# Moving TensorE's operands by 32 bytes: loaded tensors on multiples of 64, streamed ones on 32 modulo 64

## The chip, the cores and the metric

The kernel runs on one core of a Trainium2 chip. The metric is the device time of one execution in microseconds (us), median of several runs.

## The reference

Sliding-window attention with a few global keys, then two feed-forward networks over the same 1,536 tokens. All tensors are float32.

```python
# attention: batch 2, 8 heads, 768 positions, head size 64; 8 global keys, 96 local ones
keep = (key < n_global) | ((rel >= 0) & (rel < n_local))
scores = where(keep, q @ k.T / sqrt(64) - slope[h] * dist, -1e9)
x = softmax(scores) @ v                      # -> (1536, 512)
# first feed-forward network: 512 -> 1024 -> 512
h = x @ w_in
x = (layernorm(h * softmax(h)) * g_ln) @ w_out
# second one: 512 -> 1536 -> 512
xn = x / rms(x) * rms_g
out = (silu(xn @ w_gate) * (xn @ w_val)) @ w_down
```

## The kernel before

One program, five engines, every wait written out by hand with semaphores. The work has two parts.

In the first part a loop goes over 12 tiles of 128 tokens. For each tile the four head pairs are scored (`score_pair`), the probabilities are turned (`turn_pair`) and multiplied with the values (`mix_pair`). Between these the first feed-forward network of the tiles before is worked in: `turn_x`, `ffn_in`, `turn_ln`, `ffn_out`.

In the second part a loop goes over 6 blocks of 256 tokens. Each block has 12 steps, m = 0 to 11. A step is `widen` for the gate columns (12 matmuls), `widen` for the value columns (12 matmuls), and `narrow` for the step before (6 matmuls). At m = 7 and m = 10 a `turn_y` of four transposes for the next block stands between gate and value.

Each product of two float32 tensors is made of three matmuls in the type float32r, over a rounded part `_hi` and the rest `_lo` of each factor (lines 396, 397, 398, which in the trace carry all of these products):

```python
def product(pe, acc, hi, lo, other_hi, other_lo, first, last):
    pe.matmul(acc, hi, other_hi, start=first, stop=False)
    pe.matmul(acc, hi, other_lo, start=False, stop=False)
    return pe.matmul(acc, lo, other_hi, start=False, stop=last)
```

The second argument of a matmul is loaded into TensorE as weights (always 128 or 116 columns), the third is streamed through it. So `widen` loads the weight matrices `gate` and `val` and streams the activations `yt`; `narrow` loads the activations `act` and streams the matrix `down`; `ffn_in` loads `xt` and streams `in`; `ffn_out` loads `ln` and streams `out`. A transpose loads the tensor that it turns and streams `ident`. `mix_pair` loads `probs_t` and streams `v_in` in plain float32; the transposes too are plain float32. The load of one matmul goes on while the matmul before it streams.

The matrices lie in blocks of 512 columns. Blocks 0, 1 and 2 of `gate` and `val` serve the steps m = 0 to 3, 4 to 7 and 8 to 11; the blocks of `down` serve `narrow` of the same m.

Where a tensor lies: `sbuf` (line 94) takes the next address in every partition that is a multiple of 32 bytes, in the order of the calls. The first tensor, `ident`, starts at byte 16,512, a multiple of 64. Most sizes are multiples of 64 bytes, so a tensor has the residue of the one ahead of it, until a small tensor shifts it. Tensors of the second part lie over those of the first part. Added up from the shapes, the start of each tensor that TensorE reads is, modulo 64 (inside a tensor every slice that a matmul of float32r starts at, except the keys and probabilities, adds a multiple of 64):

| matmuls | loaded: residue | streamed: residue |
|---|---|---|
| `widen`, blocks 0 and 2 | gate, val: 0 | yt: 32 |
| `widen`, block 1 | gate, val: 32 | yt: 32 |
| `narrow`, block 0 | act: 32 | down: 32 |
| `narrow`, block 1 | act: 32 | down: 0 |
| `narrow`, block 2 | act: 32 | down_hi: 32, down_lo: 0 |
| `ffn_in` | xt: 0 | in: 32 |
| `ffn_out` | ln: 0 | out: 0 |
| `mix_pair` | probs_t: 32 | v_in: 32 |
| `score_pair` | queries in qk_hi: 32 | keys in qk_hi, k_lo: 32 for one head, 0 for the other |
| `turn_pair` | probs: 32, 48, 0, 16 in turn | ident: 0 |
| `turn_x`, `turn_ln` | x, gated: 0 | ident: 0 |
| `turn_y` | yn: 32 | ident: 0 |

Of the kernel before, what the change touches and what calls it, by code (L numbers as in the profile page):

```python
# [23 lines left out]
F32 = mybir.dt.float32  # L24
# [3 lines left out]
P = 128  # L28
# [6 lines left out]
FAR = 1 << 20  # L35
BATCHES = 2
SPARE = 8192
RSQRT_SEED = float(0x5F3759DF)
NEWTON = 3


def fused_kernel(nc, qk_pairs, v_windows, n_global, n_local,
# [47 lines left out]
    with whole:  # L90
        def sem(name):
            return whole.enter_context(nc.semaphore(name))

        def sbuf(ctx, name, shape, dt=F32):
            return ctx.enter_context(nc.sbuf_tensor(name, shape, dt))

        w_hi, w_lo = {}, {}

        def place(ctx, keys):
            for kind, n in keys:  # L100
                w_hi[kind, n] = sbuf(ctx, f"{kind}{n}_hi", [P, KJ, BANK], F32R)
                w_lo[kind, n] = sbuf(ctx, f"{kind}{n}_lo", [P, KJ, BANK], F32R)


        ident = sbuf(whole, "ident", [P, P])
        gln_col = sbuf(whole, "gln_col", [P, K1])
        rms_col = sbuf(whole, "rms_col", [P, KM])
# [8 lines left out]
        with ExitStack() as one:  # L116
# [4 lines left out]
            v_in = sbuf(one, "v_in", [HALF, 2, 2, model])  # L121
# [17 lines left out]
            in_front_of_spare = nc.sbuf_bytes_remaining  # L139
            spare = sbuf(one, "spare", [P, SPARE])  # L140

# [5 lines left out]
            for name, width in widths.items():  # L147
                gen[name] = spare[:, at:at + width]
                at += width
            assert at <= SPARE  # L150
            x = sbuf(one, "x", [P, heads, d])
# [19 lines left out]
        with ExitStack() as two:  # L171
            place(two, plan[OVER_ATTENTION:OVER_IN])
            y_in = sbuf(two, "y_in", [P, 2, 2, model])
            yn = sbuf(two, "yn", [P, 2, model])
            yt_hi = sbuf(two, "yt_hi", [P, 2, KM, WIDE], F32R)
            yt_lo = sbuf(two, "yt_lo", [P, 2, KM, WIDE], F32R)
            silu = sbuf(two, "silu", [P, 2, WIDE])
            act_sb = sbuf(two, "act_sb", [P, 2, WIDE])
            act_hi = sbuf(two, "act_hi", [P, 2, WIDE], F32R)
            act_lo = sbuf(two, "act_lo", [P, 2, WIDE], F32R)  # L180
            o_sb = sbuf(two, "o_sb", [P, 2, model])

            place(two, [plan[OVER_ATTENTION - 1]])
            kind, n = plan[-1]
            w_hi[plan[-1]] = sbuf(two, f"{kind}{n}_hi", [P, KJ, BANK], F32R)
            sbuf(two, "unused", [P, (nc.sbuf_bytes_remaining - in_front_of_spare) // 4])

            place(two, plan[FFN2:OVER_ATTENTION - 1])
            place(two, plan[OVER_IN:-1])
            w_lo[plan[-1]] = sbuf(two, f"{kind}{n}_lo", [P, KJ, BANK], F32R)  # L190
# [612 lines left out]
        def _(dve):  # L803
# [204 lines left out]
            def take_variance(t):  # L1008
# [13 lines left out]
                dve.wait_ge(ln_steps, at + 8)  # L1022
                nc.vector.tensor_scalar(seed_bits[:, 1:2], seed_bits[:, 0:1], -1.0, RSQRT_SEED,
                                        ALU.mult, ALU.add).then_inc(seed_ready, 1)
# [12 lines left out]
            def scale_of_y(b):  # L1037
# [3 lines left out]
                if not known(b) or b >= 1:  # L1041
# [6 lines left out]
                dve.wait_ge(rms_steps, at + 2)  # L1048
                nc.vector.tensor_scalar(rstd_bits[:, 1], rstd_bits[:, 0], -1.0, RSQRT_SEED, ALU.mult, ALU.add
                                        ).then_inc(rms_steps, 1)  # L1050
# [403 lines left out]
```

## Time and profile before

| | before |
|---|---|
| median of 3 runs | 599.11 us (598.56 to 600.3) |
| span of the profiled execution (its own time is not listed apart from it) | 596.7 us |
| TensorE matmul busy | 566.4 us, 95% |
| VectorE busy | 305.0 us, 51% |
| ScalarE busy | 258.1 us, 43% |
| mean granted TensorE clock | 0.991 |

The span goes from the first to the last instruction of one execution; the median of the runs is 2.4 us above it. Matmuls overlap in the profile: one is listed from the start of its stream to its modelled end, some 160 ns after its last column, so what a matmul costs is read from the distance between the starts of two neighbours, called the pitch here. A few per cent of the matmul records are missing, which shows as fewer matmuls than the program has.

### The profile page before, as it was taken

Reading aid. Unit: us, or ns where it says so; the run is one execution under the profiler, and the core shown is the slowest. Engines: PE = TensorE matmul, PEld = TensorE weight load, DVE = VectorE, ACT = ScalarE, POOL = GpSimd, SP = SyncE. Lnnn points to the kernel's source line nnn. Section 1 sums busy time; section 2 is a strip of 40 time slices with the busy share of each in tenths; the row PEclk is TensorE's granted clock in tenths of the full one; section 3 lists DMA queues with packets and bytes.
Section 4 is the critical chain, followed back from the end, with each engine's and each line's share of the span. In section 5 each row is a group of like instructions: output and inputs, shape, how many; then the busy total and the mean of one; then the engine's idle time right before and its main releaser. Section 6 shows DMA issues by size and latency. Waiting matters only on the chain.

```text
span 596.7 us, 10660 instructions
## 1 busy us (share of the span) xinstructions
PE 566.4 (95%) x3696; PEld 511.4 (86%) x3696; DVE 305.0 (51%) x786; ACT 258.1 (43%) x597; POOL 74.6 (13%) x215
## 2 busy tenths in 40 slices
PE   2488999999999999999999999999999999999997
PEld 1477888888888888878899999999999999999996
DVE  5478788777877898868455223222222222231211
ACT  2566756655665677646454212221222222222112
POOL 1240220222112205213010010001001000100000
PEclk9998799999999999999999999999999999999999
DMA  7676464433443343232532100010020000000000
GB/s 171 185 192 163 132 182 125 121 101 101 124 113 103 105 126 96 83 135 82 176 109 93 49 23 2 1 70 1 1 70 0 0 0 35 0 0 36 2 1 36
DMA packets 22965, 46.95 MB, mean 79 GB/s; under 512 B 4128, under 2 KB 4128, under 8 KB 22928
## 3 DMA queue, kind: packets, MB, share of 16 engines
q1 hardware_dynamic: 22928, 46.48, 26.8%
q8 instruction: 20, 0.33, 0.2%
q14 instruction: 17, 0.14, 0.1%
HBM read 40.18 MB, written 6.29 MB: 78 GB/s over the span
## 4 chain that ended last, share of the span: by engine, by line
PE 78%; DVE 9%; DMA 3%; issue 3%; POOL 3%; ACT 2%; SPq 1%; ACTq 0%; DVEq 0%
PE hidden L396 9%; PE hidden L397 8%; PE hidden L398 8%; PE mixed L1211 5%; PE mixed L396 3%; PE mixed L397 3%; PE scores_b L396 3%; PE scores_b L397 3%; PE scores_b L398 3%; PE mixed L398 3%; PE turned L396 3%; PE turned L397 3%; PE scores_a L397 3%; PE turned L398 3%; PE scores_a L396 3%
## 5 line engine op out<-in xcount | busy, mean ns | idle before, releaser
L708 ACT ACTIVATE act_hi<-act_sb 128x256 fp32r<-128x256 f32 x72 | 30.1, 418 | 108.7 <-DVE act_sb L1070 108.7
L1211 PEld LDWEIGHTS mixed<-v_in,probs_t 116*128 116x128 f32 x384 | 55.3, 210 | 14.5 <-ACT probs_t L659 10.8
L1211 PE MATMUL mixed<-v_in,probs_t 116*128 116x64 f32 x384 | 54.2, 289 | 9.8 <-ACT probs_t L659 9.8
L1070 DVE TENSOR_TENSOR act_sb<-mixed,silu 128x256 f32<-128x256 f32 x36 | 15.3, 425 | 93.7 <-PE mixed L398 93.1
L1070 DVE TENSOR_TENSOR act_sb<-turned,silu 128x256 f32<-128x256 f32 x36 | 15.3, 424 | 89.0 <-PE turned L398 86.5
L396 PE MATMUL hidden<-down_hi,act_hi 128*128 128x512 f32 x144 | 57.0, 396 | 0.1
L397 PE MATMUL hidden<-down_lo,act_hi 128*128 128x512 f32 x144 | 56.9, 395 | 0.0
L398 PE MATMUL hidden<-down_hi,act_lo 128*128 128x512 f32 x144 | 56.7, 394 | 0.0
L659 ACT ACTIVATE probs_t<-turned 116x512 f32<-116x512 f32 x48 | 28.7, 597 | 60.7 <-PE turned L1196 60.7
L1075 DVE TENSOR_TENSOR act_lo<-act_sb,act_hi 128x256 fp32r<-128x256 f32 x72 | 30.6, 425 | 34.9 <-ACT act_hi L708 34.9
L649 ACT ACTIVATE probs<-logits,neg_max 128x232 f32<-128x232 f32 x96 | 45.7, 482 | 5.8 <-DVE neg_max L961 5.8
L639 ACT ACTIVATE qk_hi<-qk_raw 128x720 fp32r<-128x720 f32 x48 | 38.1, 795 | 14.2 <-DMA qk_raw<-qk_pairs 14.2
L396 PE MATMUL hidden<-in_hi,xt_hi 128*128 128x512 f32 x96 | 42.5, 443 | 0.0
L396 PE MATMUL turned<-yt_hi,val_hi 128*128 128x256 f32 x144 | 40.8, 283 | 0.0
L396 PE MATMUL mixed<-yt_hi,val_hi 128*128 128x256 f32 x144 | 40.8, 283 | 0.0
L396 PE MATMUL scores_a<-yt_hi,gate_hi 128*128 128x256 f32 x144 | 40.4, 281 | 0.0
L397 PE MATMUL turned<-yt_lo,val_hi 128*128 128x256 f32 x144 | 40.4, 280 | 0.0
L397 PE MATMUL mixed<-yt_lo,val_hi 128*128 128x256 f32 x144 | 40.4, 280 | 0.0
L397 PE MATMUL scores_b<-yt_lo,gate_hi 128*128 128x256 f32 x144 | 40.4, 280 | 0.0
L397 PE MATMUL scores_a<-yt_lo,gate_hi 128*128 128x256 f32 x144 | 40.4, 280 | 0.0
L398 PE MATMUL turned<-yt_hi,val_lo 128*128 128x256 f32 x144 | 40.3, 280 | 0.0
L398 PE MATMUL scores_b<-yt_hi,gate_lo 128*128 128x256 f32 x144 | 40.3, 280 | 0.0
(140 smaller groups left out, 1537.2 us busy)
## 6 DMA issues: line engine op xcount, KB each, us to landing
qk_raw<-qk_pairs SPq DMA_DIRECT2D x96, 180.0 KB, 3.5
v_in<-v_windows SPq DMA_DIRECT2D x12, 464.0 KB
staging<-w_gate SPq DMA_DIRECT2D x3, 1024.0 KB, 6.5
staging<-w_val SPq DMA_DIRECT2D x3, 1024.0 KB, 5.5
y_spill<-y_out SPq DMA_DIRECT2D x12, 256.0 KB, 8.4
staging<-w_down SPq DMA_DIRECT2D x3, 1024.0 KB, 5.5
y_in<-y_spill SPq DMA_DIRECT2D x6, 512.0 KB, 3.7
out<-o_sb SPq DMA_DIRECT2D x12, 256.0 KB, 2.1
```

The source lines that it names most:

```text
L396: pe.matmul(acc, hi, other_hi, start=first, stop=False)
L397: pe.matmul(acc, hi, other_lo, start=False, stop=False)
L398: return pe.matmul(acc, lo, other_hi, start=False, stop=last)
L639: nc.scalar.activation(qk_hi[:, p % 2], qk_raw[:, p], ACT.Copy).then_inc(qk_rounded, 1)
L649: nc.scalar.activation(probs[:, p % 2, h], logits[:, 2 * (p % 2) + h], ACT.Exp, bias=neg_max[:, even, head:head + 1], scale=-1.0, accum_ou ...
L659: nc.scalar.activation(probs_t[:, p % 2], turned[0:HALF, :], ACT.Copy).then_inc(probs_t_ready, 1)
L708: nc.scalar.activation(act_hi[:, slot], act_sb[:, slot], ACT.Copy).then_inc(act_rounded, 1)
L1070: nc.vector.tensor_tensor(act_sb[:, slot], val_ps[slot][:, 0:WIDE], silu[:, slot], ALU.mult).then_inc(act_ready, 1)
L1075: nc.vector.tensor_tensor(act_lo[:, slot], act_sb[:, slot], act_hi[:, slot].bitcast(F32), ALU.subtract).then_inc(act_split, 1)
L1211: ins = pe.matmul(mixed[:, head * d:(head + 1) * d], probs_t[:, p % 2, h, half], v_in[:, even, half, head * d:(head + 1) * d], start=(half ...
```

## The change

`sbuf` puts a filler of 32 bytes ahead of a tensor, if its last dimension is 128 or more and its start would have the wrong residue. Names that begin as in `MOVED` are to start at 32 modulo 64, all others at multiples of 64. No instruction is added, removed or moved.

```diff
+SBUF_BYTES = 224 * 1024 - 32
+HALF_LINE = 32
+MOVED = ("ident", "v_in", "in0", "in1", "out0", "out1", "down", "yt_", "y_in")
...
         def sbuf(ctx, name, shape, dt=F32):
+            if shape[-1] >= P:
+                halves = (SBUF_BYTES - nc.sbuf_bytes_remaining + HALF_LINE - 1) // HALF_LINE
+                if halves % 2 != name.startswith(MOVED):
+                    ctx.enter_context(nc.sbuf_tensor(f"before_{name}", [P, HALF_LINE // 4], F32))
             return ctx.enter_context(nc.sbuf_tensor(name, shape, dt))
...
-            sbuf(two, "unused", [P, (nc.sbuf_bytes_remaining - in_front_of_spare) // 4])
+            two.enter_context(nc.sbuf_tensor("unused", [P, (nc.sbuf_bytes_remaining - in_front_of_spare) // 4], F32))
```

Seven fillers stand in the first part's list (that of `ident` included) and nine in the second's; 3,264 and 1,408 bytes of a partition stay free. The residues after it, added up in the same way:

| matmuls | loaded, streamed before | loaded, streamed after |
|---|---|---|
| `widen`, blocks 0 and 2 | 0, 32 | 0, 32 |
| `widen`, block 1 | 32, 32 | 0, 32 |
| `narrow`, block 0 | 32, 32 | 0, 32 |
| `narrow`, block 1 | 32, 0 | 0, 32 |
| `narrow`, block 2 | 32, 32 and 32, 0 | 0, 32 |
| `ffn_in` | 0, 32 | 0, 32 |
| `ffn_out` | 0, 0 | 0, 32 |
| `mix_pair` | 32, 32 | 0, 32 |
| `score_pair` | 32, 32 or 32, 0 | 0, 0 or 0, 32 |
| `turn_pair` | 32, 48, 0, 16, ident 0 | 0, 16, 32, 48, ident 32 |
| `turn_x`, `turn_ln` | 0, 0 | 0, 32 |
| `turn_y` | 32, 0 | 0, 32 |

`staging` and `qk_raw`, into which the DMAs of weights, queries and keys write, go from 32 to 0 modulo 64, as `y_out` does.

## Rows read from the trace of the kernel before

**Rows 1.** The page: span, busy time, clock by slice, chain by engine.
```profile
span 596.7 us, 10660 instructions
...
PE 566.4 (95%) x3696; PEld 511.4 (86%) x3696; DVE 305.0 (51%) x786; ACT 258.1 (43%) x597; POOL 74.6 (13%) x215
...
PEclk9998799999999999999999999999999999999999
...
PE 78%; DVE 9%; DMA 3%; issue 3%; POOL 3%; ACT 2%; SPq 1%; ACTq 0%; DVEq 0%
```

**Rows 2.** TensorE's waits, 0 to 60 us, then 60 to 290: total, times, longest.
```profile
PE scores_a L1183 <- DVE qk_hi L939: 11.1, 2, 8.5
PE mixed L1211 <- ACT probs_t L659: 9.8, 3, 8.2
...
PE turned_x L1251 <- DVE gated L1028: 0.9, 2, 0.7
```

**Rows 3.** Timeline of TensorE, first matmul of each group: start us, duration us.
```profile
502.87 0.28 PE L396 MATMUL mixed<-yt_hi,val_hi 128*128 128x256 f32 x1
...
504.27 0.40 PE L396 MATMUL hidden<-down_hi,act_hi 128*128 128x512 f32 x1
...
505.66 0.28 PE L396 MATMUL scores_a<-yt_hi,gate_hi 128*128 128x256 f32 x1
...
507.09 0.28 PE L396 MATMUL turned<-yt_hi,val_hi 128*128 128x256 f32 x1
...
508.53 0.40 PE L396 MATMUL hidden<-down_hi,act_hi 128*128 128x512 f32 x1
...
519.87 0.60 PE L1282 MATMUL turned_x<-ident,yn 128*128 128x128 f32 x4
520.22 0.36 PE L396 MATMUL mixed<-yt_hi,val_hi 128*128 128x256 f32 x1
520.42 0.28 PE L397 MATMUL mixed<-yt_lo,val_hi 128*128 128x256 f32 x1
...
521.74 0.40 PE L396 MATMUL hidden<-down_hi,act_hi 128*128 128x512 f32 x1
...
523.14 0.28 PE L396 MATMUL scores_a<-yt_hi,gate_hi 128*128 128x256 f32 x1
```

**Rows 4.** Windows over one block's steps 0 to 3, 4 to 7, 8 to 11.
```profile
488.91:505.66 16.75, 16.75 (x122) 15.70 (x121) 3.38 (x9) 4.29 (x10) 0.00 (x0) 1.00 0.08 31
505.66:523.14 17.48, 17.48 (x126) 16.43 (x124) 4.62 (x14) 3.80 (x9) 2.32 (x12) 1.00 0.00 0
523.14:540.37 17.23, 17.23 (x126) 16.15 (x125) 4.61 (x11) 3.81 (x9) 0.00 (x0) 1.00 0.00 0
```

**Rows 5.** Timeline, long runs of `ffn_in` and `ffn_out`: first and last of each.
```profile
263.32 0.39 PE L397 MATMUL hidden<-in_lo,xt_hi 128*128 128x512 f32 x1
...
265.64 0.39 PE L398 MATMUL hidden<-in_hi,xt_lo 128*128 128x512 f32 x1
...
291.83 0.39 PE L396 MATMUL y_acc<-out_hi,ln_hi 128*128 128x512 f32 x1
...
295.00 0.39 PE L398 MATMUL y_acc<-out_hi,ln_lo 128*128 128x512 f32 x1
```

**Rows 6.** Groups by form on TensorE, 66 to 262 us: busy us, mean ns.
```profile
L398 PE MATMUL hidden<-in_hi,xt_lo 128*128 128x512 f32 x79 | 31.4, 397 | 0.0
L398 PE MATMUL y_acc<-out_hi,ln_lo 128*128 128x512 f32 x79 | 31.3, 396 | 0.0
L397 PE MATMUL y_acc<-out_lo,ln_hi 128*128 128x512 f32 x79 | 30.9, 391 | 0.0
L397 PE MATMUL hidden<-in_lo,xt_hi 128*128 128x512 f32 x78 | 30.8, 394 | 0.0
L1196 PE MATMUL turned<-ident,probs 128*116 128x128 f32 x156 | 23.7, 275 | 0.0
...
L1251 PE MATMUL turned_x<-ident,gated 128*128 128x128 f32 x80 | 12.1, 273 | 0.2 <-DVE ln_lo L1033 0.2
```

**Rows 7.** Windows around the one stretch at the lower clock.
```profile
52.00:56.00 4.00, 2.60 (x20) 2.22 (x18) 3.92 (x11) 3.42 (x10) 0.00 (x0) 1.00 1.00 205
...
60.00:64.00 4.00, 4.00 (x18) 3.85 (x18) 3.24 (x13) 3.22 (x9) 2.14 (x6) 0.50 0.26 71
64.00:68.00 4.00, 4.00 (x15) 3.18 (x15) 2.64 (x6) 1.44 (x5) 1.18 (x5) 0.67 0.22 72
```

## The prediction

> **What bounds the kernel now.** I read the page first, then TensorE's waits, then the distances between starts on TensorE. The page says that TensorE is busy for 566.4 of 596.7 us and carries 78% of the chain that ended last [rows 1]. The waits say where the other 30 us are: before 60 us, where TensorE stands for queries and keys (11.1 us) and for probabilities (9.8 us). From 60 to 290 us it waits in four places for 2.1 us in all, the largest 0.9 us [rows 2]. In the second network it waits for nothing until the last step; a block's windows show it busy for all of their length [rows 4]. So from 60 us on, the time is the sum of the pitches of TensorE's matmuls. A change that adds and removes no instruction can act only through the pitch, or through the first 60 us.
>
> **The trace has the experiment in it.** In the second network, steps 0 to 3 and 8 to 11 of `widen` load from residue 0 and stream from 32, and steps 4 to 7 load from 32 and stream from 32. The instructions are otherwise the same. The value group of step 3 takes 504.27 - 502.87 = 1.40 us for 12 matmuls, 116.7 ns each. The gate group of step 4 takes 507.09 - 505.66 = 1.43 us, 119.2 ns each, and the value group of step 4 takes 508.53 - 507.09 = 1.44 us, 120.0 ns each [rows 3]. By steps: 0 to 3 take 16.75 us, 4 to 7 take 17.48 us, and 8 to 11 take 17.23 us [rows 4]. The last two hold a `turn_y` each, which costs 520.22 - 519.87 = 0.35 us, and 0.08 us more as the matmul behind it has 0.20 us to its neighbour and not 0.12 [rows 3]. Without it they are 17.05 and 16.80 us. Steps 8 to 11 are as fast as 0 to 3 within 0.05 us, at the same residues though at quite other addresses; steps 4 to 7 are slower by 0.25 to 0.30 us. I take the residues as the cause, since the load for the next matmul goes on beside the stream of this one.
>
> The Trainium skill speaks against this. Its page "SBUF — State Buffer", section "A bandwidth-pool intuition that's wrong (but worth ruling out)", gives TensorE a second, independent read port for the weight load beside that of the streamed operand. By that rule loading and streaming would not meet, and the change would be worth 0 and the time 599.1. The trace disagrees: the 120.0 against 116.7 ns above are between matmuls that differ in the loaded tensor's place alone. I keep the rule as the third rival.
>
> **The change part by part.**
>
> Block 1 of `widen` goes from 32, 32 to 0, 32, which is what blocks 0 and 2 have. Four gate groups win 0.03 us and four value groups 0.04 us each: 0.28 us in a block [rows 3], which agrees with the windows' 0.25 to 0.30 [rows 4]. Six blocks: 6 x 0.28 = -1.7 us. This is the firm term; its bounds are the windows' 1.5 and 1.8.
>
> Blocks of `narrow`, 432 matmuls that stream 512 columns, all come to 0, 32. Before, six of block 0 (32, 32) took 505.66 - 504.27 = 1.39 us and six of block 1 (32, 0) took 523.14 - 521.74 = 1.40 us [rows 3], 231.7 and 233.3 ns each. The rows nearest to the new pairing are those of `ffn_in`, which has 0, 32 at this width: in its long run the pitch is (265.64 - 263.32) / 10 = 232.0 ns [rows 5]. So blocks 1 and 2 stay, and block 0 loses about 0.01 us for six: 24 groups, +0.2 us. The bounds: all 432 at the best pitch seen at this width, 226.4 ns (next paragraph), would give 432 x 5.5 = -2.4 us; twice the loss between the pairings, 3 ns on 432, +1.3 us.
>
> `ffn_out` goes from 0, 0 to 0, 32 and has 288 matmuls. Here the old pairing looks like the better one. Its long run, behind a few that settle, has a pitch of (295.00 - 291.83) / 14 = 226.4 ns, while `ffn_in` at 0, 32 stays at 232.0 [rows 5]. Forty-eight matmuls stand in three long runs, of which I count some 35 as settled: 35 x 5.6 = +0.2 us. The other 240 stand in runs of six between other work. There the durations of the second and third matmul of a product are 391 and 396 ns against 394 and 397 ns for `ffn_in`, 2 ns apart in the mean [rows 6]. The first matmul of a product can't be compared, as what stands ahead of the run differs. First and last of a run are set by their neighbours, so 160 count: 160 x 2 = +0.3 us. Bounds for all of `ffn_out`: 0 if the rise is due to something else about `ffn_in`, and 288 x 5.6 = +1.6 us.
>
> `mix_pair` goes from 32, 32 to 0, 32, 384 matmuls in plain float32. No row has it at another pairing. The step that `widen` shows, 3.3 ns, would be 384 x 3.3 = 1.3 us either way. I take 0: the nearest rows are those of plain float32 too, the transposes. They show 273 ns with `gated` and `ident` both at 0, and 275 ns with `probs` at four different residues [rows 6]. At such a mix any effect of the size of `widen`'s would show.
>
> For the same reason `turn_x`, `turn_ln` and `turn_y` count nothing. `ffn_in` and blocks 0 and 2 of `widen` keep their residues. `score_pair` and `turn_pair` keep the difference between loaded and streamed, since both move by 32. If not the difference but the absolute residue counted, their 192 and 192 matmuls could move by 3.3 ns, 1.3 us either way; I take 0.
>
> DVE, ACT and POOL work and the DMAs now meet tensors at other residues. They are hidden by TensorE from 60 us on, since it waits for 2.1 us in 230 [rows 2]. Their cover is gone only before 60 us, where TensorE stood for over 20 us [rows 2]. If `qk_raw` and `staging` at multiples of 64 made the loading and rounding 2% quicker or slower, that would be 0.4 us; I take 0. The fillers cost bytes alone.
>
> The sum is -1.7 + 0.2 + 0.2 + 0.3 = -1.0 us, on the span of 596.7 us: 595.7 us. The median of the runs stands 2.4 us above the span; carried over, that is 598.1 us. The change is 0.17%, and 0.3% (1.8 us) is about what a measurement of this kernel can tell from no change. So most of the likeliest case ends as no measurable change, with the sign of a gain.
>
> **The rivals.**
>
> First: the 512-column matmuls gain too. What would speak for it is that 226 ns do occur at this width; against it, that they occur at equal residues, and `ffn_in` has the new pairing and 232 ns. If all of `narrow` came to 226.4 ns, the time would be 599.1 - 1.7 - 2.4 = 595.0 us; if half of it did, 596.2. Chance 0.18.
>
> Second, on the other side: they lose more than `ffn_in` shows. 432 + 288 = 720 matmuls stand against the gain of 1.7 us. From 1.7 / 720 = 2.4 ns each on, the kernel is slower than before; from 4.9 ns on, measurably. At the 5.6 ns between the two long runs [rows 5] the time is 599.1 - 1.7 + 4.0 = 601.4 us. For it: that gap is real and I apply it to 35 matmuls only. Against it: block 1 of `narrow` already is at 233.3 ns, the slow end. Chance 0.10.
>
> Third: the residues do nothing, and steps 4 to 7 are slow for another reason of those addresses. The time stays at 599.1 us. Chance 0.10.
>
> Fourth: the clock. TensorE's granted clock falls to 0.50, which is 1.2 GHz, after a stretch in which it was busy for 2.60 of 4 us, and is back at 2.4 GHz within 64 to 68 us [rows 7]. Some 10 us of work at half speed cost about 5 us. A shift of a fraction of a microsecond in the waits before 60 us could take this away (594 us by -1.0 and -4.5) or lengthen it (up to 603 us). Nothing in the change aims at it. Chance 0.10, half on each side.
>
> **How the numbers follow.** The likeliest case has 0.52, with a range of its own from 597.0 to 599.1 us by the bounds above and a scatter of half a microsecond. Faster by over 0.3% is below 597.3 us: 0.17 of the first rival, 0.05 of the fourth, 0.09 of the likeliest case: 0.31. Slower by over 0.3% is above 600.9 us: 0.07 of the second rival, 0.05 of the fourth: 0.12. Within 0.3%: 0.57. The range goes from 595.5 us, which takes in most of the first rival, to 600.0 us, and leaves out the two clock cases, the bulk of the second rival and the best end of the first.
>
> **What would show it.** In the profile after, the second third of a block should be as long as the last, 17.2 us, with the value groups of steps 4 to 7 at 1.40 us; if they stay at 1.44, the third rival holds. The six matmuls of `narrow` should take 1.39 to 1.40 us everywhere; 1.36 speaks for the first rival, 1.42 for the second. The long run of `ffn_out` should go from 226 to about 232 ns. `mix_pair` and the transposes should keep their durations. The prediction is wrong if `mix_pair` or the scores move by some nanoseconds, or if the lower clock covers another stretch than before.

## The result, and the profile after

The changed kernel takes 600.63 us (median of 22 runs, 598.98 to 602.18), the kernel before 599.06 us (22 runs): a ratio of 1.0027, 95% interval 1.0019 to 1.0035. It is slower by 1.6 us, where a gain of 1.0 us was forecast, and 600.63 lies above the range.

The page of the changed kernel answers to [rows 1]:

```profile
span 598.7 us, 10660 instructions
...
PE 568.8 (95%) x3696; PEld 513.3 (86%) x3696; DVE 305.1 (51%) x786; ACT 258.1 (43%) x597; POOL 74.5 (12%) x215
...
PEclk9998799999999999999999999999999999999999
...
PE 81%; DVE 8%; issue 3%; POOL 3%; DMA 3%; ACT 1%; SPq 1%; ACTq 0%; DVEq 0%
```

Everything but TensorE is as it was: VectorE 305.1 against 305.0 us, ScalarE the same, the clock digits the same. TensorE is busy 2.4 us longer with the same 3,696 matmuls. Its waits answer to [rows 2], 0 to 60 us and then 60 to 290, and are within 0.4 us of those before:

```profile
PE scores_a L1190 <- DVE qk_hi L946: 10.9, 2, 8.4
PE mixed L1218 <- ACT probs_t L666: 9.9, 3, 8.3
...
PE turned_x L1258 <- DVE gated L1035: 0.5, 1, 0.5
```

So matmuls have become slower by their pitch. The windows over a block's steps 0 to 3, 4 to 7 and 8 to 11 answer to [rows 4]. All 12 steps of a block now follow the rule of the change:

```profile
490.26:507.18 16.92, 16.92 (x121) 15.86 (x120) 3.40 (x9) 4.29 (x10) 0.00 (x0) 1.00 0.08 31
507.18:524.69 17.51, 17.51 (x126) 16.44 (x125) 4.62 (x14) 3.80 (x9) 2.33 (x12) 1.00 0.00 0
524.69:542.08 17.39, 17.39 (x126) 16.31 (x125) 4.60 (x11) 3.81 (x9) 0.00 (x0) 1.00 0.00 0
```

Steps 4 to 7, which were to win 0.28 us, take 17.51 us against 17.48. Steps 0 to 3 and 8 to 11, whose residues modulo 64 did not change, take 16.92 against 16.75 and 17.39 against 17.23. The block is 0.36 us longer. The groups' first matmuls, to be read against [rows 3], show the same:

```profile
504.37 0.28 PE L403 MATMUL mixed<-yt_hi,val_hi 128*128 128x256 f32 x1
...
505.79 0.40 PE L403 MATMUL hidden<-down_hi,act_hi 128*128 128x512 f32 x1
...
507.18 0.28 PE L403 MATMUL scores_a<-yt_hi,gate_hi 128*128 128x256 f32 x1
...
508.62 0.28 PE L403 MATMUL turned<-yt_hi,val_hi 128*128 128x256 f32 x1
...
510.06 0.39 PE L403 MATMUL hidden<-down_hi,act_hi 128*128 128x512 f32 x1
```

The value group of step 3 takes 1.42 us where it took 1.40; gate and value of step 4 take 1.44 and 1.44 us, so block 1 of the matrices is still at 120 ns. The timeline from the first `widen` matmul to the end is 598.7 - 277.0 = 321.7 us against 596.7 - 276.8 = 319.9 us. These 1.8 us in one trace of each kernel cover the 1.6 us of the medians, so the loss is in the second network. The first matmul of `widen` starts within 0.2 us of where it did.

The terms on 512 columns came close to what the prediction said. The long run of `ffn_out`, first and last matmul, answers to [rows 5]; the groups of the first network, 66 to 262 us, answer to [rows 6]:

```profile
291.95 0.40 PE L403 MATMUL y_acc<-out_hi,ln_hi 128*128 128x512 f32 x1
...
295.22 0.40 PE L405 MATMUL y_acc<-out_hi,ln_lo 128*128 128x512 f32 x1
```

```profile
L1218 PE MATMUL mixed<-v_in,probs_t 116*128 116x64 f32 x312 | 39.0, 268 | 0.0
...
L404 PE MATMUL y_acc<-out_lo,ln_hi 128*128 128x512 f32 x79 | 31.2, 395 | 0.0
L405 PE MATMUL y_acc<-out_hi,ln_lo 128*128 128x512 f32 x79 | 31.2, 394 | 0.0
...
L1203 PE MATMUL turned<-ident,probs 128*116 128x128 f32 x156 | 23.8, 275 | 0.0
```

The pitch of the long run is (295.22 - 291.95) / 14 = 233.6 ns, from 226.4. The transposes are unchanged at 275 ns.

### The profile page after: what moved, and what is told of

It is laid out like the page before. It is cut to its first block, busy times and chain, and to the rows that moved or that the text cites. A ratio compares the mean times of both kernels' runs of the same rounds, so it can differ in the third digit from the quotient of the medians.

```text
span 598.7 us, 10660 instructions
## 1 busy us (share of the span) xinstructions
PE 568.8 (95%) x3696; PEld 513.3 (86%) x3696; DVE 305.1 (51%) x786; ACT 258.1 (43%) x597; POOL 74.5 (12%) x215
## 4 chain that ended last, share of the span: by engine, by line
PE 81%; DVE 8%; issue 3%; POOL 3%; DMA 3%; ACT 1%; SPq 1%; ACTq 0%; DVEq 0%
PE hidden L403 9%; PE hidden L404 9%; PE hidden L405 9%; PE mixed L1218 5%; PE turned L403 3%; PE mixed L403 3%; PE scores_b L405 3%; PE scores_a L403 3%; PE scores_b L404 3%; PE scores_b L403 3%; PE scores_a L405 3%; PE scores_a L404 3%; PE mixed L404 3%; PE turned L404 3%; PE mixed L405 3%
## 5 line engine op out<-in xcount | busy, mean ns | idle before, releaser
L403 PE MATMUL scores_b<-yt_hi,gate_hi 128*128 128x256 f32 x144 | 40.5, 281 | 0.0
```

## The experiments

In kernels of the whole computation the second network's stretch (first `widen` matmul to the end of the span) is compared between single traces. Within one trace it repeats: the four blocks between the first and the last take 51.46 us each in the kernel before. What lies before it does not: in eight traces the first `widen` matmul starts between 275.1 and 278.3 us, with no order that follows the edits.

**Pairs of addresses.** A kernel that holds one tensor of zeros over nearly all of a partition and runs groups of 16 equal matmuls. In short form:

```python
for load, stream, n in cases:        # 8 x 8 residues in 256 bytes, at two regions; the load in steps of 8192
    for i in range(16):
        pe.matmul(ps[:, 0:n], big[:, load:load + 128], big[:, stream:stream + n], start=True, stop=True)
```

> A kernel of its own that leaves out the whole computation and stores a constant: 210 groups of 16 equal float32r matmuls, each group with one place of the loaded operand and one of the streamed operand, 256 or 512 columns streamed. It asks which property of the two addresses sets the pitch. Theory A (residues modulo 64, on which the prediction rests): at 256 columns the pitch is 116.7 ns wherever the load is at 0 and the stream at 32 modulo 64, and 120.0 ns at equal residues, at every distance. Theory B (regions: block 1 of the gate and value matrices stayed at 120 ns although its residue was changed, and it is the only block that lies in the lower part of a partition as the streamed tensor does): the pitch is 120 ns when load and stream lie in the same region of the partition and some 117 ns when not, whatever the residues. Theory C: the distance of the two addresses modulo a larger power of two counts, so that the 64 pairs over 256 bytes show several levels.

The timeline of this kernel, one row for a group, with the load at a multiple of 256. Shown are the stream at 0 and 32, and at 192 and 224 modulo 256. The distance of two starts over 16 is the pitch, the first matmuls of a group included:

```profile
38.99 2.08 PE L61 MATMUL even<-big 128*128 128x256 f32 x16
40.90 2.05 PE L61 MATMUL odd<-big 128*128 128x256 f32 x16
...
50.36 1.99 PE L61 MATMUL even<-big 128*128 128x256 f32 x16
52.19 2.05 PE L61 MATMUL odd<-big 128*128 128x256 f32 x16
```

Distance 0 takes 1.91 us and distance 192 takes 1.83. Over all 210 groups the pitch, without the first five matmuls of each, goes mainly by one number, the distance from loaded to streamed operand modulo 256 bytes. The table has the means:

| distance mod 256 | 0 | 32 | 64 | 96 | 128 | 160 | 192 | 224 |
|---|---|---|---|---|---|---|---|---|
| 256 columns, ns (16 groups each, 41 at 64 and 96) | 120.0 | 117.7 | 117.8 | 119.4 | 118.7 | 117.5 | 113.9 | 117.8 |
| 512 columns, ns (2 to 8 groups each) | 227.1 | 233.5 | 229.1 | 233.1 | not run | 234.0 | 233.3 | 233.3 |

Theory A falls: distances 32 and 96, both reachable with 0 and 32 modulo 64, give 117.7 and 119.4. Theory B falls: the load in 25 places from byte 16,672 to 213,280 gives 117.8 or 117.9 (distance 64) at every one. Four distances have groups that stand apart from the rest: at 192 two of the 16 kept 117.8 ns and the others have 113.3 or 113.4; at 32 two have 116.6 and the others 117.8 or 117.9; at 160 two have 118.7 and the others 117.3 or 117.4; at 96 they lie between 119.1 and 120.2. So one distance can have two pitches, which comes back below.

With this table the two kernels' addresses can be read anew. The distances from loaded to streamed operand, modulo 256, from the same sums that gave the residues:

| | before | changed |
|---|---|---|
| `widen`, block 0 | 32 | 224 |
| `widen`, block 1 | 0 | 96 |
| `widen`, block 2 | 32 | 160 |
| `narrow`, blocks 0, 1, 2 | 0; 224; 0 and 224 | 32; 32; 32 and 96 |
| `ffn_in` | 32 | 160 |
| `ffn_out` | 0 | 32 |

The means do not give the loss by themselves. Block 0 of `widen` goes from distance 32 to 224 and block 2 from 32 to 160, which in the table is 117.7 to 117.8 and 117.7 to 117.5 ns. In the two kernels it is 116.7 to some 118.2 ns in both: at 32 the kernel before has the lower of the two pitches seen above, at 160 the changed kernel is near the higher one.

**A uniform shift.** The kernel before with 32 bytes ahead of everything.

```diff
+        whole.enter_context(nc.sbuf_tensor("shift", [P, 8], F32))
         ident = sbuf(whole, "ident", [P, P])
```

> The kernel before with one filler of 32 bytes ahead of all tensors, so that every address is 32 higher and every distance between two tensors is as before. If only the distance between loaded and streamed operand counts (theories A in its difference form, B, C) the pitches of all groups of the second network stay within 0.2 ns and the span stays at 596.7 us within 0.5. If the absolute residue counts, the pitches of the fast groups (116.7 ns) change by more than 1 ns.

Measured: one run, 599.85 us beside 596.89 us, span 598.0; the span missed the expected 596.7. The second network does not: its windows are those of [rows 4] to 0.01 us.

```profile
490.30:507.05 16.75, 16.75 (x122) 15.70 (x120) 3.39 (x9) 4.29 (x10) 0.00 (x0) 1.00 0.08 31
507.05:524.53 17.48, 17.48 (x125) 16.43 (x124) 4.63 (x14) 3.80 (x9) 2.35 (x12) 1.00 0.00 0
524.53:541.76 17.23, 17.23 (x125) 16.15 (x124) 4.61 (x11) 3.81 (x9) 0.00 (x0) 1.00 0.00 0
```

Here every tensor has the other residue modulo 64, and no third of a block moved. So the absolute residue does not count here; a rule on the difference, modulo 64 or 256, is not touched by this run. The 1.4 us more of span lie ahead of the first `widen` matmul, which starts at 278.2 us and not at 276.8.

**The distance in fine steps, and in a product's order.**

```python
for n in (256, 512):
    for d in range(0, 256, 4): group(load, stream + d, n)      # 24 matmuls each
# then steps of 64 up to 1024; a product's three terms over four slices; 232 columns; plain float32
```

> A kernel of its own that leaves out the computation, with groups of 24 equal matmuls again. Theory D, formed from the first such kernel: the pitch is a function of the distance from the loaded to the streamed operand modulo 256 bytes, and of nothing else about the addresses (256 columns: 0 gives 120.0 ns, 32 and 64 117.7, 96 119.4, 128 118.7, 160 117.5, 192 113.4, 224 117.8; 512 columns: 0 gives 226.7, 64 229.1, others 233 to 234). This one steps the distance by 4 bytes, goes past 256 in steps of 64, runs the real order of a product over four slices, and takes 232 columns and plain float32 too. Theory D says that distances 256 apart agree within 0.3 ns, that the product's order gives the same numbers as equal matmuls within 1 ns, and that plain float32 shows steps below 1 ns. Its rival E: the order of hi and lo parts matters, and the product's order is flat.

Measured, without the first eight matmuls of a group: distances 256 apart agree within 0.1 ns. The product's order gives 120.0, 117.8, 117.8, 120.2, 118.7, 117.3, 113.3, 118.3 ns at 256 columns for distances 0 to 224, within 1 ns of the first table. Plain float32 has 111.7 ns at every distance and width from one record to the next; a plain float32 matmul of the program leaves two records. 232 columns of float32r have 111.5 to 112.2 ns. So E falls, and D holds for the period of 256 bytes. D in its strict form, that nothing else counts, does not hold: this one kernel has distance 32 at 116.7, 116.9 and 117.8 ns, and 160 at 117.3 and 118.7, in groups with other groups ahead of them. The fine steps show no smooth curve. Groups of distance 12, 16, 20 and 24 on the timeline:

```profile
48.34 2.96 PE L63 MATMUL odd<-big 128*128 128x256 f32 x24
51.15 2.88 PE L63 MATMUL even<-big 128*128 128x256 f32 x24
53.86 3.10 PE L63 MATMUL odd<-big 128*128 128x256 f32 x24
56.79 3.04 PE L63 MATMUL even<-big 128*128 128x256 f32 x24
```

Distance 16 settles at 113.3 ns and distance 20, four bytes on, at 122.3. The lowest are 113.3 ns at 16, 112, 144 and 192 for 256 columns, and 226.7 ns at 28, 60, 156, 236, 240 and 252 for 512 columns.

**The same rule, another distance.** In this run and in the other runs of the whole computation below, `sbuf` takes a start modulo 256 from a table. Here the rule of the change holds in all float32r products, with distance 32 everywhere.

```diff
+            for start, residue in PLACES:
+                if name.startswith(start):
+                    at = (SBUF_BYTES - nc.sbuf_bytes_remaining + 31) // 32 * 32
+                    if (residue - at) % 256:
+                        ctx.enter_context(nc.sbuf_tensor(f"before_{name}", [P, (residue - at) % 256 // 4], F32))
+                    break
...
+PLACES = (("gate", 0), ("val", 0), ("spare", 0), ("yt_", 32), ("act_hi", 0), ("act_lo", 0), ("down", 32),
+          ("xt_", 64), ("in0", 96), ("in1", 96), ("ln_", 64), ("out0", 96), ("out1", 96))
```

> Keeps the rule of the changed kernel (tensors that are loaded at multiples of 64, those that are streamed at 32 modulo 64, in all float32r products) and sets the distance from loaded to streamed to 32 modulo 256 everywhere; the changed kernel has 224, 96 and 160 in the three blocks of the widening matmuls and 32 to 160 elsewhere. Theory D: all gate and value groups come to 116.6 to 117.7 ns, against 118.2, 120.0 and 118.2 in the changed kernel, the 512-column ones stay at 233; so the time is 1.7 to 3.6 us below the changed kernel's, 597.0 to 599.0 us, the same as before or slightly below it. Theory A (the residues modulo 64 alone): the same time as the changed kernel, 600.6 us.

Measured: 598.03 us against 598.88 for the kernel before, ratio 0.9983 (0.9970 to 0.9996); the second network's stretch is 318.9 us, 2.8 us below the changed kernel's and 1.0 below before. The gate and value groups of all steps are at 116.7 ns. The changed kernel differs from this one in its distances and not in the rule, so the rule modulo 64 is not what decides. For block 0 the comparison is closest: modulo 256 gate, val, act and down lie as in the changed kernel, and only yt is elsewhere (32, not 224). The groups go from 118.2 to 116.7 ns.

**Block 1 alone.** The prediction's first term by itself: gate and val of block 1 at 64 modulo 256 with yt kept at 96, all other distances of the float32r products as before. (`yn`, which `turn_y` loads, moves along by 32 bytes; its four transposes take 0.36 us as before.)

```diff
+PLACES = (("gate1", 64), ("val1", 64), ("yt_", 96), ("act_hi", 96), ("act_lo", 96), ("down0", 96),
+          ... ("down1", 64), ...
```

> The kernel before with one thing changed: block 1 of gate and val starts 32 bytes before the streamed tensor modulo 256 (it started at the same residue), which also is 0 and 32 modulo 64. All other distances are as before. This is the first term of the prediction by itself. Theory D: the gate and value groups of steps 4 to 7 go from 1425 to 1440 ns to 1400, the second network's stretch from 319.9 to 318.1 us, the time by 1.7 us (0.28%) below that of before. Theory A expects the same, but cannot say why the changed kernel, which has the same residues modulo 64, did not show it.

Measured: 597.24 us against 598.53, ratio 0.9977 (0.9963 to 0.9990). The windows over a block:

```profile
489.38:506.14 16.76, 16.76 (x122) 15.70 (x120) 3.40 (x9) 4.30 (x10) 0.00 (x0) 1.00 0.08 31
506.14:523.38 17.24, 17.24 (x125) 16.16 (x124) 4.61 (x14) 3.81 (x9) 2.35 (x12) 1.00 0.00 0
523.38:540.61 17.23, 17.23 (x126) 16.14 (x124) 4.62 (x11) 3.81 (x9) 0.00 (x0) 1.00 0.00 0
```

Steps 4 to 7 are now as long as 8 to 11. They win 0.24 us a block, 1.4 us in six blocks; the stretch is 318.4 us, 1.5 below before.

**Distance 192 and 0.** The best multiples of 32 in the table.

```diff
+PLACES = (("gate", 0), ("val", 0), ("spare", 0), ("yt_", 192), ("act_hi", 192), ("act_lo", 192), ("down", 192),
+          ("xt_", 96), ("in0", 96), ("in1", 96), ("ln_", 96), ("out0", 96), ("out1", 96))
```

> Distance 192 modulo 256 for the widening matmuls (256 columns) and 0 for all that stream 512 columns. Theory D: widening pitch 113.4 ns instead of 117.8 in the mean before, 1728 x 4.4 = 7.6 us less; narrowing 432 matmuls from 232.2 to some 229 ns (runs of six don't settle), 1.3 us less; the first network's inner 512-column matmuls of xt from 232.8 to 231, 0.5 us less: in all 9 us less than before, 590 us. If history matters more than the distance, the gain is smaller, down to 2 us. Theory A says no more than 2 us either way, since the loaded tensors lie at 0, 192 and 96 modulo 256 and the streamed ones at 192 and 96.

Measured: 598.08 us against 598.88, ratio 0.9989 (0.9976 to 1.0002); the 9 us did not come. The stretch is 319.2 us. All `narrow` groups fell to 1,387 ns as expected, but nearly all gate and value groups are at 117.8 ns. In two kinds of places they were faster. The value groups behind a `turn_y` take 1,464 to 1,470 ns with the 92 ns that the transposes cost them, so 1,372 to 1,378 or some 114.5 ns a matmul. And in steps 0 to 3 of the first block, where `ffn_out` or transposes run ahead of the gate group and not `narrow`, the gate and value groups take 1,359 to 1,361 ns, 113.3 a matmul, but for the one right behind transposes (1,458). The first matmuls of step 3's gate, value and `narrow` group and of step 4's gate and value group:

```profile
293.43 0.28 PE L404 MATMUL scores_b<-yt_hi,gate_hi 128*128 128x256 f32 x1
...
294.79 0.28 PE L404 MATMUL mixed<-yt_hi,val_hi 128*128 128x256 f32 x1
...
296.15 0.40 PE L404 MATMUL hidden<-down_hi,act_hi 128*128 128x512 f32 x1
...
297.53 0.28 PE L404 MATMUL scores_a<-yt_hi,gate_hi 128*128 128x256 f32 x1
...
298.95 0.28 PE L404 MATMUL turned<-yt_hi,val_hi 128*128 128x256 f32 x1
```

Behind `ffn_out` (ln and out at 96) the gate group takes 1.36 us, behind `narrow` (act and down at 192) 1.42 us. The same pair of places runs at 117.8 or at about 113 ns, by what stood ahead.

**Whole steps.** Three steps of 12 + 12 + 6 matmuls for each of 70 sets (distance of `widen`; act's place; distance of `narrow`).

> A kernel of its own that leaves out the computation: steps of the second network as TensorE sees them, 12 + 12 widening matmuls and 6 narrowing ones in the real order, three times for each of 70 sets of distances. In the run with distance 192 the widening groups behind a narrowing group came to 117.8 ns, and those behind a transpose to some 114, although equal matmuls alone had given 113.3. Theory F: at some distances TensorE has two steady patterns, and what stands ahead decides which one it falls into; then among 16, 112, 144 and 192 some hold 113.3 ns behind a narrowing group and a step takes about 24 x 113.3 + 6 x 230 = 4.10 us, against 4.18 to 4.20 at 32. Rival: behind a narrowing group none of them does, and no step is below 4.15 us.

Measured: a step takes from 4.08 to 4.27 us. The first matmuls of one step's groups, for (192; act 0; 0) and then for (192; act 96; 0):

```profile
746.42 0.28 PE L52 MATMUL gate_ps<-big 128*128 128x256 f32 x1
...
747.84 0.28 PE L52 MATMUL val_ps<-big 128*128 128x256 f32 x1
...
749.25 0.39 PE L52 MATMUL down_ps<-big 128*128 128x512 f32 x1
...
834.12 0.28 PE L52 MATMUL gate_ps<-big 128*128 128x256 f32 x1
...
835.48 0.28 PE L52 MATMUL val_ps<-big 128*128 128x256 f32 x1
...
836.85 0.39 PE L52 MATMUL down_ps<-big 128*128 128x512 f32 x1
...
838.24 0.28 PE L52 MATMUL gate_ps<-big 128*128 128x256 f32 x1
```

The distances within each product are the same in both. With act at 0 the gate group takes 1.42 us, with act at 96 it takes 1.36. So the distance within a product allows more than one pattern, and what stands ahead chooses: F holds and its rival falls. It is not always the group just ahead alone. At (144; 0; 32) the third step's gate group takes 1.36 us and the second's 1.43, both behind a `narrow` group of 1.40 us at the same places modulo 256. The shortest step, 4.08 us, is at (144; 0; 252), with 1,360 ns for each of the three groups.

**The two sets that the steps kernel points to.**

```diff
-PLACES = (... ("act_hi", 192), ("act_lo", 192), ("down", 192), ...)
+PLACES = (... ("act_hi", 96), ("act_lo", 96), ("down", 96), ...)
```

> As the run with distance 192, with act and down at 96 instead of 192 modulo 256: all distances within a product stay (192 and 0), only that between the two kinds of work differs. Theory F (two steady patterns, chosen by what stands ahead), by the groups of the steps kernel (1359, 1370, 1384 ns): a step without a transpose takes 4.11 us instead of 4.21, 72 steps are 7 us less than before, so about 591.5 us. Theory D alone (the distance within a product is all): no difference to the run with distance 192, 598.1 us.

Measured: 592.71 us against 598.53, ratio 0.9895 (0.9877 to 0.9914). The stretch is 313.2 us, 6.7 us below before. The gate groups are at 1,359 ns, the value groups at 1,370, the `narrow` groups at 1,384: the steps kernel's numbers to the nanosecond. Windows over a block, steps 0 to 3, 4 to 7, 8 to 11:

```profile
485.81:502.26 16.45, 16.45 (x122) 15.41 (x120) 3.40 (x9) 4.30 (x10) 0.00 (x0) 1.00 0.08 32
502.26:519.17 16.91, 16.91 (x126) 15.88 (x125) 4.61 (x14) 3.80 (x9) 2.35 (x12) 1.00 0.00 0
519.17:536.07 16.90, 16.90 (x125) 15.87 (x124) 4.60 (x11) 3.80 (x9) 0.00 (x0) 1.00 0.00 0
```

For the other set yt and down are views that begin four and seven words inside a tensor:

```diff
+            yt = sbuf(two, "yt", [P, 8 + 4 * KM * WIDE], F32R)              # at 128 modulo 256
+            yt_hi, yt_lo = (yt[:, at:at + 2 * KM * WIDE].rearrange("p (e k n) -> p e k n", e=2, k=KM)
+                            for at in (4, 4 + 2 * KM * WIDE))
...
+                    both = sbuf(ctx, f"{kind}{n}", [P, 8 + 2 * KJ * BANK], F32R)        # at 224, views from word 7
```

> Distance 144 for the widening matmuls and 252 for the narrowing ones, with act at 0: yt starts 16 bytes and down 28 bytes off a multiple of 32, by views into larger tensors. In the steps kernel every group held 1360 ns, 4.08 us a step. If the pattern survives the transposes and the first step of a block, 72 steps are 9.6 us less than before, some 589 us; if each transpose throws it into the other pattern (1425 ns) for the rest of the block, the gain falls to about 3 us.

Measured: 590.63 us against 598.53, ratio 0.986 (0.984 to 0.988). The stretch is 311.8 us, 8.1 below before. This is the fastest version, 10.0 us below the changed kernel in the medians, which stem from different sets of runs:

```profile
484.24:500.56 16.32, 16.32 (x121) 15.37 (x120) 3.40 (x9) 4.30 (x10) 0.00 (x0) 1.00 0.08 32
500.56:517.40 16.84, 16.84 (x125) 15.88 (x124) 4.64 (x14) 3.81 (x9) 2.35 (x12) 1.00 0.00 0
```

Steps 0 to 3 take 4 x 4.08 us. Steps 4 to 7 hold a `turn_y` and take 0.52 us more, where before it cost 0.43: some of the pattern is lost behind a transpose, but not for the rest of the block. In steps 0 to 3 of the first block, behind `ffn_out` at 96 with distance 0, the gate and value groups take 1.42 to 1.43 us; the steps kernel has 1.43 for (144; 96; 0) too.

**Own load or next load.** Does a stream meet the load of the next matmul, or is it the matmul's own pair that counts?

In short form:

```python
for i in range(24):
    a, b = load + apart * (i % 2), stream + apart * (i % 2)        # apart = 0, 128, 64, 4096 bytes
```

> A kernel of its own that leaves out the computation. Every second matmul has both operands 128 bytes further on, so a matmul's own distance d stays, while the distance between its stream and the load of the next matmul, which goes on beside that stream, is d + 128. If the meeting of a stream with the next load sets the pitch, as the prediction had it (G), own distance 128 now gives at 512 columns what 0 gave with equal places, 226.7 ns, and own distance 0 gives 233.6. If the own distance sets it (H), 0 stays at 226.7 and 128 at 233.6. Moves by 4096 bytes must change nothing; moves by 64 give alternating neighbours of d + 64 and d - 64.

Measured, by the timeline: at 512 columns own distances 0 and 128, first with equal places and then with every second matmul 128 bytes on. Each row and the next one stand 24 matmuls apart:

```profile
39.05 5.60 PE L48 MATMUL even<-big 128*128 128x512 f32 x24
44.49 5.77 PE L48 MATMUL odd<-big 128*128 128x512 f32 x24
...
83.63 5.84 PE L48 MATMUL even<-big 128*128 128x512 f32 x24
89.31 5.69 PE L48 MATMUL odd<-big 128*128 128x512 f32 x24
...
105.97 5.69 PE L48 MATMUL even<-big 128*128 128x512 f32 x24
111.49 5.68 PE L48 MATMUL odd<-big 128*128 128x512 f32 x24
```

Own distance 0 goes from 226.7 to (89.31 - 83.63) / 24 = 236.7 ns when its neighbours are 128 bytes on, so the own distance alone does not set the pitch: H falls. Own distance 128 with neighbours at distance 0 gives (111.49 - 105.97) / 24 = 230.0 and not 226.7: G in its simple form falls too. At 256 columns the same moves take own distance 192 from 113.3 to 116.7 ns and own distance 0 from 120.0 to 118.0. Moves by 4,096 bytes change nothing. That places of neighbouring matmuls act on each other is shown; by which rule is open.

## Why the prediction was wrong

**The step that failed.** "I take the residues as the cause": 0 and 32 modulo 64 was read from [rows 3, 4] as the fast pairing. What the rows had in them was distance 32 against distance 0, modulo 256. Both descriptions fit the kernel before, since blocks 0 and 2 happen to have the same distance. The change keeps the first and gives up the second. The changed kernel's block 1 shows it, still at 120 ns with residues 0 and 32, and so does the run with the same rule at distance 32 (2.8 us less in the second network than the changed kernel). The uniform shift (residues swapped, windows the same) takes away the absolute residues as well. The prediction had the warning before it and passed it by: with the addresses summed up, "at quite other addresses" could have been checked against more moduli than 64.

**Block 1 of `widen`, -1.7 us.** In the changed kernel its distance is 96, and 17.51 us against 17.48 is a change of 0.2 us in six blocks the other way. The gain itself can be had: at distance 32 the same steps gave 1.4 us of the 1.7 forecast.

**Blocks 0 and 2 of `widen`, 0.** The prediction said that they keep their residues and so their time. Their distances went from 32 to 224 and 160, and their windows lost 0.17 + 0.16 us a block, nearly all of it in the gate and value groups: six blocks, +2.0 us, of which the first block, where `ffn_out`, transposes and one wait stand between the steps, gives back some 0.2. This term is the result. It was not bounded at all, though the text asked what an absolute residue could do to the scores. For block 0 the run with distance 32 shows that the place of yt alone makes the difference. For block 2 the place of gate and val against act changed together with the distance, and no run takes the two apart; the pair tables alone would have it gain.

**`narrow`, +0.2 us.** The twelve groups of a block sum to 16.74 us against 16.72, so +0.1 us. The direction holds, and the size to 0.1 us.

**`ffn_out`, +0.2 and +0.3 us.** The long run went to 233.6 ns (232 forecast). The second and third matmuls of a product went from 391 and 396 to 395 and 394 ns, 1 ns in the mean and not 2: about 0.2 us. `ffn_in` of the kernel before was the right row to read this from, since it has distance 32, to which `ffn_out` came. That `ffn_in` itself went to 160 did no harm, as the pair kernel has 233.5 and 234.0 ns for 32 and 160; this was luck, since the prediction took it for unchanged.

**`mix_pair`, transposes, scores, 0.** Held: `mix_pair` stayed at 268 ns and the transposes at 275. The run in fine steps agrees: plain float32 matmuls have 111.7 ns a record at every distance, 232 columns of float32r stay within 0.7 ns. The transposes were not run by themselves. The prediction's 384 matmuls of `mix_pair` are records, two for each of 192 matmuls.

**The first 60 us, 0, and the clock.** Held. The waits are the same within 0.2 us, and the granted clock is 0.50 from 60 to 64 us and 0.65 from 64 to 68, against 0.50 and 0.67.

**The rivals.** The first (512-column matmuls gain) was wrong. The third was half right: steps 4 to 7 were slow for another property of their addresses than the residue, as it said, and its sign, value groups still at 1.44 us, came true; that nothing else would move, so 599.1 us, was wrong. The second ended on the right side with the wrong place: the loss is in the 256-column matmuls. The rule that load and stream use independent ports, which the prediction weighed from the Trainium skill's page "SBUF — State Buffer", section "A bandwidth-pool intuition that's wrong (but worth ruling out)", remains contradicted as far as time goes: 113.3 to 123.1 ns for the same matmul by its operands' places. No run shows whether it is at the ports that the two meet.

## What to carry to other kernels

Where TensorE is the bound and the matmuls are of float32r, the places of loaded and streamed operand are worth up to 1.4% here, with no instruction changed; what counts is their distance modulo 256 bytes and what ran ahead. A small kernel that runs the real order of loads and streams at several places found the two best sets here, and its numbers came back within 2 ns a group behind the first block, in the steps without a transpose. A table of single pairs promised 9 us, of which 0.8 came. A natural experiment in a trace with two cases proves a difference, not its description: before building on "residue modulo 64", list every property that the two cases differ in, and ask which of them the change keeps. In a kernel whose matmuls have no slack, a tensor moved by 32 bytes for another reason can cost or give a microsecond or two (1.6 us lost here), so compare such edits with the distances held.

## What the runs showed of the hardware

- The pitch of float32r matmuls at 2.4 GHz depends on the distance from loaded to streamed operand modulo 256 bytes: 113.3 to 123.1 ns at 256 columns, 226.7 to 240.0 ns at 512. Four bytes more can cost 9 ns (113.3 at 16, 122.3 at 20).
- Plain float32 matmuls of 64 and 128 columns have 111.7 ns from record to record, two records a matmul, at all eight distances.
- One distance can have more than one steady pitch: 113.3 and 117.8 ns at 192, 116.6 and 117.8 at 32, 117.3 and 118.7 at 160. At 192 and 144 (113.3 or 119) what stands ahead chooses.
- The region of the partition does not matter (25 places), nor does a shift of all tensors together.
- Open: why 256 bytes, how far back what stands ahead still counts, and how neighbouring matmuls at different distances act on each other (226.7 to 236.7 ns by moving every second pair 128 bytes).
